# Attention and two expert stages on one core: block sums of the first two pairs by TensorE, two buffers for raw keys and queries, the other sums in three chunks on GpSimd

## Chip, core and metric

The kernel runs on one core of one Trainium2 chip. The metric is the device time of one execution in microseconds (us), as the median of several runs. Before the change it is 567.54 us (three runs, 567.53 to 567.76).

## What is computed

```python
# attention: B, H, S, D = 2, 8, 768, 64
block, window = (32, 16)
k_sum = k.reshape(B, H, nb, block, D).max(axis=3)      # nb = 24 blocks
v_sum = v.reshape(B, H, nb, block, D).mean(axis=3)
scores_l = scale * q @ k.T, kept where |i - j| < window
scores_s = scale * q @ k_sum.T + log(block)
a = softmax(concat([scores_l, scores_s], -1))
attn = a @ concat([v, v_sum])
# x = attn rows (1536 x 512); each row goes to one of 8 experts
out1[mask] = gate_w[mask, None] * (np.maximum(x[mask] @ w1[e], 0.0) @ w2[e])
# and then through a second layer
h = np.maximum(out1 @ w_in, 0.0)
out = h * h @ w_out
```

The change touches only the way to `v_sum` and the buffers of raw keys and queries. `v_sum` is 24 block means of the values for each of the 16 heads.

## The kernel before

The program is written for each engine by itself; the order in each engine's queue is the order in the text, and the engines meet by counting semaphores. Attention goes by pairs of heads: eight pairs, written as (it, par) with pair = 2 it + par. A pair's 768 queries are cut into 12 windows of 64 (SUBS); each window sees 94 near keys (NEAR) and the 24 block sums. A pair is done in two halves, g = 0 and 1, and the text numbers them n = 2 pair + g.

For one pair, SyncE loads raw keys and queries (`load_qk`, line 347) into `k_raw` and `q_raw`, a single buffer each, after the previous pair's were regrouped. VectorE regroups keys (`regroup_k`, 1326), ScalarE queries (`regroup_q`, 1099). TensorE turns them in three parts (`fill`, 701), the other engines move them out of PSUM (`move_k`, `move_kq`, `move_q`), VectorE takes the maximum of the key blocks (`key_max`) and TensorE makes the scores (`scores`, 715, 723, 730). ScalarE takes exponentials (`exps`, 1110). TensorE turns the probabilities (`turn_probs`, 743) and multiplies them with the value tile `v_win` (`values`, 763). `pair_step` on each engine (TensorE 781, ScalarE 1124, VectorE 1374) writes out how these interleave: while one pair is finished, the next one is scored and the one after that is turned.

A value tile `v_win` has 120 rows for each of the 12 windows: 94 near rows, loaded by `load_near` (361; six small-row DMAs on SyncE, 363, 364, 366), two unused ones and, in rows 96 to 119, the 24 block means, the same for all 12 windows. There are four tiles: 0 and 1 for even and odd pairs, 2 and 3 for the last two pairs. Their constant parts are cleared once: tiles 0 and 1 by VectorE (1445 to 1449), 2 and 3 by GpSimd (528 to 532).

The means come from `v_blk`, the values as 384 rows (one a block) of 32 x 64 in three chunks of 128 rows. The first chunk serves pairs 0, 1 and part of 2; half of it is added up by GpSimd (519), the other by VectorE (`sum_blocks`, 1431). SyncE stores its sums to `mean_dram` (391), waits, and loads them with a broadcast over the 12 windows into tiles 0 and 1 (378). Chunks 1 and 2 are added up by GpSimd (564, 567), which stores them itself (568). For pairs 2 to 7 SyncE loads the means into window 0 alone (373) and GpSimd copies them to the other eleven (599), counted by `means_spread`; it does that after its chunks and after its small constants (570 to 585).

After the pairs come the routing, gathers by GpSimd, the experts (`three`, lines 915 to 917) and the second layer (the same lines), all ordered behind the attention.

## Time and profile before

| | |
|---|---|
| median of three runs | 567.54 us |
| the profiled execution | 567.62 us |
| its span, first to last instruction | 565.9 us |
| mean granted TensorE clock | 0.969 |
| TensorE busy | 526.7 us, 93% |
| VectorE busy | 275.9 us, 49% |
| ScalarE busy | 236.0 us, 42% |
| GpSimd busy | 94.5 us, 17% |
| chain that ended last, by engine | PE 80%, DMA 5%, SPq 4%, DVE 4%, ACT 3% |

The profile is of one execution. PE is TensorE, PEld its weight loads, DVE VectorE, ACT ScalarE, POOL GpSimd, SPq the queue of SyncE. A busy share is a mean over stages with different limits. The chain is followed back from the last instruction, at each step to what released it; it says which work set the end. "issue" is time in which an engine waited for nothing that the profile shows. Helpers make several instructions share one line.

### The profile page before, as it was taken

Reading aid. Unit: us, or ns where it says so; the run is one execution under the profiler, and the core shown is the slowest. Engines: PE = TensorE matmul, PEld = TensorE weight load, DVE = VectorE, ACT = ScalarE, POOL = GpSimd, SP = SyncE. Lnnn points to the kernel's source line nnn. Section 1 sums busy time; section 2 is a strip of 40 time slices with the busy share of each in tenths; the row PEclk is TensorE's granted clock in tenths of the full one; section 3 lists DMA queues with packets and bytes.
Section 4 is the critical chain, followed back from the end, with each engine's and each line's share of the span. In section 5 each row is a group of like instructions: output and inputs, shape, how many; then the busy total and the mean of one; then the engine's idle time right before and its main releaser. Section 6 shows DMA issues by size and latency. Waiting matters only on the chain.

```text
span 565.9 us, 10958 instructions
## 1 busy us (share of the span) xinstructions
PE 526.7 (93%) x4442; PEld 475.2 (84%) x4442; DVE 275.9 (49%) x439; ACT 236.0 (42%) x416; POOL 94.5 (17%) x123
## 2 busy tenths in 40 slices
PE   5599987599999995999999999999999999999997
PEld 4487776598998985898989999889989999999995
DVE  7577867567675877465483232223223233222221
ACT  5478757455666652444452222223123222222221
POOL 5771111102653057211010000000000000000000
PEclk9689989699999999899999999999999999999999
DMA  6955776965769857385420020002002002000000
GB/s 204 273 165 153 188 205 215 294 230 164 284 223 350 287 182 259 131 286 190 175 76 0 1 75 1 0 13 62 0 0 74 0 0 74 0 0 37 2 2 37
DMA packets 62655, 69.50 MB, mean 123 GB/s; under 512 B 22512, under 2 KB 47088, under 8 KB 62232
## 3 DMA queue, kind: packets, MB, share of 16 engines
q1 hardware_dynamic: 59160, 57.36, 31.9%
q0 software_dynamic: 3456, 11.60, 6.0%
q8 instruction: 27, 0.44, 0.3%
q14 instruction: 12, 0.10, 0.1%
HBM read 58.88 MB, written 10.06 MB: 122 GB/s over the span
## 4 chain that ended last, share of the span: by engine, by line
PE 80%; DMA 5%; SPq 4%; DVE 4%; ACT 3%; issue 2%; POOL 2%; POOLq 0%; ACTq 0%; DVEq 0%
PE psum L915 24%; PE psum L916 23%; PE psum L917 23%; PE psum L701 1%; DMA k_raw<-in_k 1%; DMA x_rows_sb<-x_rows,gather_tab 1%; SPq L364 1%; PE psum L743 1%; PE psum L909 1%; DMA x_rows_sb<-x_rows,idx_g 1%; SPq L363 1%; PE psum L723 1%; PE psum L1018 1%; PE psum L763 1%; ACT prob L1110 1%
## 5 line engine op out<-in xcount | busy, mean ns | idle before, releaser
L917 PE MATMUL psum<-x_hi,win_lo 128*128 128x256 f32 x384 | 108.7, 283 | 0.0
L916 PE MATMUL psum<-x_lo,win_hi 128*128 128x256 f32 x384 | 108.7, 283 | 0.0
L915 PE MATMUL psum<-x_hi,win_hi 128*128 128x256 f32 x384 | 108.5, 282 | 0.0
L1722 DVE TENSOR_TENSOR h_sq<-h_relu 128x512 f32<-128x512 f32 x48 | 33.2, 693 | 126.5 <-ACT h_relu L1291 126.5
L915 PE MATMUL psum<-wb_hi,h_hi 128*128 128x512 f32 x208 | 83.2, 400 | 0.0
L1291 ACT ACTIVATE h_relu<-psum 128x512 f32<-128x512 f32 x48 | 28.7, 598 | 127.3 <-PE psum L917 127.3
L916 PE MATMUL psum<-wb_lo,h_hi 128*128 128x512 f32 x208 | 81.6, 392 | 0.0
L917 PE MATMUL psum<-wb_hi,h_lo 128*128 128x512 f32 x208 | 81.6, 392 | 0.0
L915 PEld LDWEIGHTS psum<-x_hi,win_hi 128*128 128x128 f32 x384 | 73.6, 192 | 1.4
L916 PEld LDWEIGHTS psum<-x_lo,win_hi 128*128 128x128 f32 x384 | 73.6, 192 | 1.4
L917 PEld LDWEIGHTS psum<-x_hi,win_lo 128*128 128x128 f32 x384 | 73.6, 192 | 0.0
L915 PE MATMUL psum<-x_hi,wa_hi 128*128 128x256 f32 x224 | 64.7, 289 | 0.6 <-DVE x_lo L1635 0.6
L916 PE MATMUL psum<-x_lo,wa_hi 128*128 128x256 f32 x224 | 64.1, 286 | 0.0
L917 PE MATMUL psum<-x_hi,wa_lo 128*128 128x256 f32 x224 | 64.1, 286 | 0.0
L1624 DVE TENSOR_TENSOR wa_lo<-w_raw,wa_hi 128x1024 fp32r<-128x1024 f32 x32 | 41.1, 1342 | 36.0 <-ACT wa_hi L1204 36.0
L1725 DVE TENSOR_TENSOR h_lo<-h_sq,h_hi 128x512 fp32r<-128x512 f32 x48 | 33.3, 693 | 33.0 <-ACT h_hi L1296 33.0
L917 PEld LDWEIGHTS psum<-wb_hi,h_lo 128*128 128x128 f32 x208 | 39.3, 189 | 8.5
L1296 ACT CAST h_hi<-h_sq 128x512 fp32r<-128x512 f32 x48 | 29.8, 620 | 40.0 <-DVE h_sq L1722 40.0
L915 PEld LDWEIGHTS psum<-wb_hi,h_hi 128*128 128x128 f32 x208 | 39.6, 190 | 7.6 <-issue 0.2
L916 PEld LDWEIGHTS psum<-wb_lo,h_hi 128*128 128x128 f32 x208 | 39.6, 190 | 7.3
L915 PEld LDWEIGHTS psum<-x_hi,wa_hi 128*128 128x128 f32 x224 | 43.7, 195 | 1.5 <-issue 1.2
L916 PEld LDWEIGHTS psum<-x_lo,wa_hi 128*128 128x128 f32 x224 | 43.8, 195 | 0.2
(211 smaller groups left out, 886.6 us busy)
## 6 DMA issues: line engine op xcount, KB each, us to landing
w_raw<-in_moe_w SPq DMA_DIRECT2D x56, 512.0 KB, 6.1
win_raw<-in_moe_w_in POOLq DMA_DIRECT2D x8, 512.0 KB, 7.2
w_raw<-in_moe_w_out SPq DMA_DIRECT2D x8, 512.0 KB, 4.8
k_raw<-in_k SPq DMA_DIRECT2D x8, 384.0 KB, 4.3
q_raw<-in_q SPq DMA_DIRECT2D x8, 384.0 KB, 4.6
v_blk<-in_v SPq DMA_DIRECT2D x3, 1024.0 KB, 7.5
v_win<-in_v SPq DMA_DIRECT2D x16, 192.0 KB, 3.5
x_rows<-x_all SPq DMA_DIRECT2D x8, 384.0 KB, 5.8
```

The source lines that it names most:

```text
L363: sp.dma_start(dst[PAD:PAD + QS, :, hh, 0:D], src[:, 0, :, :]).then_inc(v_loaded[slot], 16)
L364: sp.dma_start(dst[0:PAD, 1:SUBS, hh, 0:D], src[QS - PAD:QS, 0, 0:SUBS - 1, :])\
L701: mm = pe.transpose(psum[:, bank, n * P:(n + 1) * P], side[:, j, :, :].rearrange("p h d -> p (h d)"), ident[:, :])
L723: pe.matmul(ps_score[g][QS * s:QS * s + QS, hh, t, 0:SUM0], q_t[par][h0:h0 + D, i * QS:(i + 1) * QS], k_t[par][h0:h0 + D, i * QS:i * QS + ...
L915: pe.matmul(o, l_hi, r_hi, start=start, stop=False)
L916: pe.matmul(o, l_hi, r_lo, start=False, stop=False)
L917: return pe.matmul(o, l_lo, r_hi, start=False, stop=stop)
L1291: act.activation(h_relu[c % 2][:, :], ps_h[:, c % 4, :], ACT.Relu).then_inc(relu_made, 1)
L1296: act.copy(h2_hi[c % 3][:, :, :].rearrange("p f t -> p (f t)"), h_sq[c % 2][:, :])\
L1624: dve.tensor_tensor(lo[:, at:at + PIECE], w_raw[:, c, :], hi[:, at:at + PIECE], ALU.subtract)\
L1722: dve.tensor_tensor(h_sq[c % 2][:, :], h_relu[c % 2][:, :], h_relu[c % 2][:, :], ALU.mult)\
L1725: dve.tensor_tensor(h2_lo[c % 3][:, :, :].rearrange("p f t -> p (f t)"), h_sq[c % 2][:, :], h2_hi[c % 3][:, :, :].rearrange("p f t -> p (f ...
```

## The change

For pairs 0 and 1 TensorE makes the block sums from the near rows of the value tile: `sum_means` multiplies, window by window, a matrix `picks` of zeros and ones with the 94 near rows and adds the 12 products up in PSUM; VectorE copies the 24 sums into window 0 of the tile (`place_means`), and GpSimd copies them to the others, as it does for later pairs. The other six pairs' sums are made by GpSimd alone in three chunks of 96 rows (VB), the first of them between the spreads of pairs 0 and 1. The broadcast load is gone. GpSimd also clears tile 1 and regroups the keys of pair 1. Raw keys and queries have a second buffer, in the place of `x_all` slots that are written late. The order at the start of each engine's program is changed to match; all products with values now wait for their own pair's `means_spread`.

```diff
         v_heads = v.rearrange("b h (i r) d -> r (b h) i d", r=QS)
-        v_blocks = v.rearrange("b h (n t) d -> (b h n) (t d)", t=BLOCK).rearrange("(c p) x -> p c x", p=P)
+        v_blocks = v.rearrange("b h (n t) d -> (b h n) (t d)", t=BLOCK).rearrange("(c p) x -> p c x", p=VB)
...
+        def raw(pair):
+            if pair % 2 == 0:
+                return k_raw[:, :, :, :], q_raw[:, :, :, :]
+            return [x_all[:, i, :, :].rearrange("p t c -> p (t c)").rearrange("p (h j d) -> p h j d", h=2, j=TILES)
+                    for i in (PAIRS - 1, PAIRS - 2)]
...
             def load_qk(pair):
-                for dst, src, loaded, copied in ((k_raw, k_heads, k_loaded, k_regrouped),
-                                                 (q_raw, q_heads, q_loaded, q_regrouped)):
-                    if not (isinstance(pair, int) and pair == 0):
-                        sp.wait_ge(copied, pair)
-                    sp.dma_start(dst[:, :, :, :].rearrange("p h j d -> p h (j d)"),
-                                 src[:, bass.ds(2 * pair, 2), :]).then_inc(loaded, 16)
+                for dst, src, loaded, copied in ((raw(pair)[0], k_heads, k_loaded, k_regrouped),
+                                                 (raw(pair)[1], q_heads, q_loaded, q_regrouped)):
+                    if pair >= 2:
+                        sp.wait_ge(copied, pair - 1)
+                    sp.dma_start(dst.rearrange("p h j d -> p h (j d)"),
+                                 src[:, bass.ds(2 * pair, 2), :]).then_inc(loaded[pair % 2], 16)
...
                 slot = v_slot(it, par)
-                if it > 0:
-                    sp.dma_start(v_win[slot][SUM0:COLS, 0, :, 0:D], mean_heads[:, 4 * it + 2 * par:4 * it + 2 * par + 2, :])\
-                      .then_inc(means_loaded[slot], 16)
-                    return
-                for hh in range(2):
-                    mean = mean_heads[:, bass.ds(4 * it + 2 * par + hh, 1), :]
-                    sp.dma_start(v_win[slot][SUM0:COLS, :, hh, 0:D], mean.broadcast_to([NSUM, SUBS, D]))\
-                      .then_inc(v_loaded[slot], 16)
+                sp.dma_start(v_win[slot][SUM0:COLS, 0, :, 0:D], mean_heads[:, 4 * it + 2 * par:4 * it + 2 * par + 2, :])\
+                  .then_inc(means_loaded[slot], 16)
+            def load_blocks(c):
+                sp.dma_start(v_blk[0:VB, c - 1, :], v_blocks[:, c, :]).then_inc(vb_loaded[c - 1], 16)
             sp.dma_start(emb_sb[:, :], emb).then_inc(emb_loaded, 16)
             load_qk(0)
-            sp.dma_start(v_blk[:, 0, :], v_blocks[:, 0, :]).then_inc(vb_loaded[0], 16)
-            sp.dma_start(tau_sb[:, 0:1], tau.broadcast_to([P, 1])).then_inc(tau_loaded, 16)
+            load_qk(1)
             sp.wait_ge(zeros_made, 1)
             load_near(0, 0, free=True)
-            load_qk(1)
-            sp.wait_ge(zeros_made, 2)
+            sp.dma_start(tau_sb[:, 0:1], tau.broadcast_to([P, 1])).then_inc(tau_loaded, 16)
+            load_qk(2)
+            sp.wait_ge(late_zeros_made, 1)
             load_near(0, 1, free=True)
-            sp.wait_ge(mean_made, 1)
-            sp.dma_start(mean_dram[0:P, :], v_mean[:, 0, :]).then_inc(means_stored[0], 16)
-            sp.dma_start(v_blk[:, 1, :], v_blocks[:, 1, :]).then_inc(vb_loaded[1], 16)
-            sp.wait_ge(means_stored[0], 16)
-            load_means(0, 0)
-            load_means(0, 1)
-            load_qk(2)
-            sp.dma_start(v_blk[:, 2, :], v_blocks[:, 2, :]).then_inc(vb_loaded[2], 16)
+            load_blocks(1)
             load_qk(3)
-            sp.wait_ge(late_zeros_made, 1)
-            sp.wait_ge(means_stored[1], 16)
+            load_blocks(2)
             for it in range(1, PAIRS // 2 - 1):
                 for par in range(2):
                     load_near(it, par)
-                    if it == 1 and par == 1:
-                        sp.wait_ge(means_stored[2], 16)
+                    sp.wait_ge(means_stored[it - 1], 16)
                     load_means(it, par)
                     load_qk(2 * it + 2 + par)
+                    if it == 1 and par == 0:
+                        load_blocks(3)
+            sp.wait_ge(late_zeros_made, 3)
+            sp.wait_ge(means_stored[PAIRS // 2 - 2], 16)
             for par in range(2):
                 load_near(PAIRS // 2 - 1, par, free=True)
                 load_means(PAIRS // 2 - 1, par)
...
-            pool.wait_ge(vb_loaded[0], 16)
+            after(pool.memset(picks[:, :], 0.0))
+            pick = picks[:, SUBS * 2:SUBS * 2 + 2]
+            after(pool.memset(pick, 1.0))
+            after(pool.affine_select(out=pick, in_=pick, compare_op=ALU.is_ge, fill=0.0, base=-PAD,
+                                     pattern=[[-BLOCK, 2]], channel_multiplier=1))
+            pool.affine_select(out=pick, in_=pick, compare_op=ALU.is_ge, fill=0.0, base=PAD + BLOCK - 1,
+                               pattern=[[BLOCK, 2]], channel_multiplier=-1).then_inc(picks_made, 1)
+            pool.wait_ge(picks_made, 1)
             pool.wait_ge(consts_made, 1)
-            at = BLOCK * D // 2
-            width = at // 2
-            while width >= D:
-                last = pool.tensor_tensor(v_blk[:, 0, at:at + width], v_blk[:, 0, at:at + width],
-                                          v_blk[:, 0, at + width:at + 2 * width], ALU.add)
-                if width > D:
-                    after(last)
-                width //= 2
-            last.then_inc(half_summed, 1)
-            pool.wait_ge(half_summed, 1)
-            for i in range(2, 4):
+            pool.wait_ge(k_regrouped, 1)
+            pool.wait_ge(k_loaded[1], 16)
+            pool.sem_inc(pool_waited, 1)
+            pool.tensor_copy(k_side[1][:, :, :, :].rearrange("p j h d -> p h j d"), raw(1)[0]).then_inc(k_regrouped, 1)
+            pool.wait_ge(k_regrouped, 2)
+            def zero_windows(i):
                 pool.memset(v_win[i][:, 0, :, :], 0.0)
                 after(pool.memset(v_win[i][:, SUBS - 1, :, :], 0.0))
                 after(pool.memset(v_win[i][QS:SUM0, :, :, :], 0.0))
                 after(pool.memset(v_win[i][0:SUM0, :, :, D:D + 1], 1.0))
                 after(pool.memset(v_win[i][SUM0:COLS, :, :, D:D + 1], float(BLOCK)))
-            pool.sem_inc(late_zeros_made, 1)
+                pool.sem_inc(late_zeros_made, 1)
+            def sum_blocks(c):
+                pool.wait_ge(vb_loaded[c], 16)
+                pool.sem_inc(pool_waited, 1)
+                width = BLOCK * D // 2
+                while width > D:
+                    after(pool.tensor_tensor(v_blk[0:VB, c, 0:width], v_blk[0:VB, c, 0:width],
+                                             v_blk[0:VB, c, width:2 * width], ALU.add))
+                    width //= 2
+                after(pool.tensor_tensor(v_mean[0:VB, c, :], v_blk[0:VB, c, 0:D], v_blk[0:VB, c, D:2 * D], ALU.add))
+                pool.dma_start(mean_dram[(c + 1) * VB:(c + 2) * VB, :], v_mean[0:VB, c, :])\
+                    .then_inc(means_stored[c], 16)
+            def spread(at):
+                pool.tensor_copy(v_win[at][SUM0:COLS, 1:SUBS, :, 0:D],
+                                 v_win[at][SUM0:COLS, 0:1, :, 0:D].broadcast_to([NSUM, SUBS - 1, 2, D]))\
+                    .then_inc(means_spread, 1)
+            zero_windows(1)
+            pool.wait_ge(means_placed, 1)
+            spread(0)
+            pool.wait_ge(means_spread, 1)
+            sum_blocks(0)
+            pool.wait_ge(means_placed, 2)
+            spread(1)
+            pool.wait_ge(means_spread, 2)
+            zero_windows(2)
+            zero_windows(3)
...
             for c in (1, 2):
-                pool.wait_ge(vb_loaded[c], 16)
-                width = BLOCK * D // 2
-                while width > D:
-                    after(pool.tensor_tensor(v_blk[:, c, 0:width], v_blk[:, c, 0:width],
-                                             v_blk[:, c, width:2 * width], ALU.add))
-                    width //= 2
-                after(pool.tensor_tensor(v_mean[:, c, :], v_blk[:, c, 0:D], v_blk[:, c, D:2 * D], ALU.add))
-                pool.dma_start(mean_dram[c * P:(c + 1) * P, :], v_mean[:, c, :]).then_inc(means_stored[c], 16)
+                sum_blocks(c)
...
-                    if 2 * it + par > 2:
-                        pool.wait_ge(means_spread, 2 * it + par - 2)
-                        end_waits()
+                    pool.wait_ge(means_spread, 2 * it + par)
+                    end_waits()
                     pool.wait_ge(means_loaded[at], 16 if at > 1 else 16 * it)
-                    pool.tensor_copy(v_win[at][SUM0:COLS, 1:SUBS, :, 0:D],
-                                     v_win[at][SUM0:COLS, 0:1, :, 0:D].broadcast_to([NSUM, SUBS - 1, 2, D]))\
-                        .then_inc(means_spread, 1)
+                    spread(at)
...
-            def fill(it, par, f, bank=7, first=False):
+            def fill(it, par, f, bank=7):
                 pair = 2 * it + par
                 if f == 0:
                     pe.wait_ge(k_regrouped, pair + 1)
-                    if not first:
+                    if pair > 0:
                         pe.wait_ge(qk_moved_act, 2 * pair)
                 elif f == 1:
                     pe.wait_ge(q_regrouped, pair + 1)
-                    if not first:
+                    if pair == 1:
+                        pe.wait_ge(emb_moved, 1)
+                    elif pair > 1:
                         pe.wait_ge(qk_moved_act, 2 * pair + 1)
-                elif not first:
+                elif pair == 1:
+                    pe.wait_ge(qk_moved_act, 3)
+                elif pair > 1:
                     pe.wait_ge(qk_moved_dve, pair + 1)
                 tiles = [("k", j) for j in range(TILES)] + [("q", j) for j in range(TILES)]
...
             def values(it, par, g):
                 n = 2 * (2 * it + par) + g
-                if isinstance(n, int) and n == 0:
-                    pe.wait_ge(emb_moved, 1)
                 if g == 0:
                     last_two = v_slot(it, par) > 1
-                    pe.wait_ge(v_loaded[v_slot(it, par)], 96 if last_two else 128 + 96 * it)
-                    if it > 0:
-                        pe.wait_ge(means_spread, 2 * it + par - 1)
+                    pe.wait_ge(v_loaded[v_slot(it, par)], 96 if last_two else 96 * it + 96)
+                    pe.wait_ge(means_spread, 2 * it + par + 1)
...
+            def sum_means(par, bank):
+                pe.wait_ge(v_loaded[par], 96)
+                for i in range(SUBS):
+                    mm = pe.matmul(ps_mean(bank), picks[:, 2 * (SUBS - i):2 * (SUBS - i) + EP],
+                                   v_win[par][0:NEAR, i, :, 0:D], start=(i == 0), stop=(i == SUBS - 1))
+                mm.then_inc(means_summed, 1)
...
                 if pair > 0:
                     turn_pair(pair - 1)
+                else:
+                    sum_means(1, 4)
                 if fills:
                     fill(it + 1, par, 1)
                 if pair > 0:
                     wait_turned(pair)
+                else:
+                    pe.wait_ge(means_placed, 2)
                 turn_probs(it, par, 1)
...
             pe.wait_ge(consts_made, 1)
             scores(0, 0, 0, first=True)
+            fill(0, 1, 0)
+            fill(0, 1, 1, bank=6)
             scores(0, 0, 1, first=True)
-            for f in range(3):
-                fill(0, 1, f)
+            fill(0, 1, 2)
+            pe.wait_ge(picks_made, 1)
+            pe.wait_ge(qk_moved_dve, 2)
+            sum_means(0, 6)
             pair_step(0, 0, True)
...
             move_k(0, 0, first=True)
             move_q(0, 0, bank=5)
-            exps(0, 0, 0, first=True)
             regroup_q(0, 1, first=True)
             move_k(0, 1, first=True)
+            exps(0, 0, 0, first=True)
             move_q(0, 1)
             pair_step(0, 0, True, first=True)
...
+                else:
+                    place_means(1, 4)
                 if fills:
                     move_kq(it + 1, par)
...
+            def place_means(par, bank):
+                dve.wait_ge(means_summed, par + 1)
+                dve.tensor_copy(v_win[par][SUM0:COLS, 0, :, 0:D],
+                                ps_mean(bank)[0:NSUM, :].rearrange("p (h d) -> p h d", h=2)).then_inc(means_placed, 1)
+            dve.memset(v_win[0][:, 0, :, 0:D], 0.0)
+            dve.memset(v_win[0][:, SUBS - 1, :, 0:D], 0.0)
+            dve.memset(v_win[0][QS:SUM0, 1:SUBS - 1, :, 0:D], 0.0)
+            dve.memset(v_win[0][0:SUM0, :, :, D:D + 1], 1.0)
+            dve.memset(v_win[0][SUM0:COLS, :, :, D:D + 1], float(BLOCK)).then_inc(zeros_made, 1)
+            embeddings()
             regroup_k(0, 0, first=True)
-            embeddings()
             move_kq(0, 0, first=True, bank=4)
...
             row_max(0, 0, 1)
-            regroup_k(0, 1, first=True)
-            move_kq(0, 1, first=True)
             key_max(0, 1)
+            place_means(0, 6)
             pair_step(0, 0, True, between=invert_tau)
             pair_step(0, 1, True)
             pair_step(1, 0, True)
```

## Rows read from the trace of the kernel before

**Rows 1.** The page, part 1: busy us (share of the span) xinstructions.

```profile
PE 526.7 (93%) x4442; PEld 475.2 (84%) x4442; DVE 275.9 (49%) x439; ACT 236.0 (42%) x416; POOL 94.5 (17%) x123
```

**Rows 2.** Chain of waits, 0 to 90 us: start us, length us, what.

```profile
17.38 2.03 DMA mean_rows<-v_mean
...
39.47 3.02 DMA k_raw<-in_k
...
46.26 0.99 ACT k_t L1082
...
52.65 0.90 issue
...
59.14 0.58 PE psum L701 x4
...
76.98 1.08 PE psum L701 x4
```

**Rows 3.** Timeline of GpSimd: start, length (us), line, operation, count [idle before <- releaser].

```profile
6.20 0.11 POOL L512 MEMSET mask<- 128x15 bf16 x1
11.07 3.38 POOL L519 TENSOR_TENSOR v_blk<-v_blk 128x512 f32<-128x512 f32 x4 [4.77 <-DMA v_blk<-in_v]
14.52 0.23 POOL L528 MEMSET v_win<- 120x160 f32 x1
...
19.62 0.13 POOL L531 MEMSET v_win<- 96x24 f32 x1
19.81 0.13 POOL L532 MEMSET v_win<- 24x24 f32 x1
23.12 5.24 POOL L564 TENSOR_TENSOR v_blk<-v_blk 128x1024 f32<-128x1024 f32 x4 [3.18 <-DMA v_blk<-in_v]
...
29.83 5.09 POOL L564 TENSOR_TENSOR v_blk<-v_blk 128x1024 f32<-128x1024 f32 x4
35.00 0.32 POOL L567 TENSOR_TENSOR v_mean<-v_blk 128x64 f32<-128x64 f32 x1
...
36.54 0.22 POOL L570 MEMSET ones<- 128x128 f32 x1
...
38.11 0.25 POOL L585 TENSOR_SCALAR_AFFINE_SELECT before<-id_e 48x48 f32<-48x48 f32 x1
41.30 1.36 POOL L599 COPY v_win<-v_win 24x1408 f32<-24x1408 f32 x1 [2.94 <-DMA v_win<-mean_rows]
49.26 1.36 POOL L599 COPY v_win<-v_win 24x1408 f32<-24x1408 f32 x1 [6.60 <-DMA v_win<-mean_rows]
```

**Rows 4.** Timeline of TensorE, 0 to 90 us.

```profile
17.14 1.11 PE L701 MATMUL psum<-ident,k_side 128*128 128x128 f32 x4 [5.52 <-DVE k_side L1326]
...
27.88 0.92 PE L763 MATMUL psum<-v_win,prob_t 120*64 120x65 f32 x24
...
37.07 0.92 PE L763 MATMUL psum<-v_win,prob_t 120*64 120x65 f32 x24
...
45.20 0.92 PE L763 MATMUL psum<-v_win,prob_t 120*64 120x65 f32 x24
...
50.24 0.92 PE L763 MATMUL psum<-v_win,prob_t 120*64 120x65 f32 x24
...
54.81 0.92 PE L763 MATMUL psum<-v_win,prob_t 120*64 120x65 f32 x24
```

**Rows 5.** Timeline of the queue of SyncE.

```profile
7.60 3.13 SPq L364 DMA_DIRECT2D v_win<-in_v  x1
...
12.20 1.56 SPq L363 DMA_DIRECT2D v_win<-in_v  x1
...
17.83 0.43 SPq L392 DMA_DIRECT2D v_blk<-in_v  x1
```

**Rows 6.** Timeline of VectorE, 0 to 90 us.

```profile
51.58 0.56 DVE L1326 COPY k_side<-k_raw 128x768 f32<-128x768 f32 x1 [1.19 <-DMA k_raw<-in_k]
```

**Rows 7.** Busy time by stretch; PEclk (granted clock) stands before the DMA share.

```profile
77.00:80.40 3.40, 3.40 (x46) 3.05 (x46) 2.10 (x4) 1.66 (x7) 1.36 (x1) 0.51 0.94 278
```

More of the change, by code:

```diff
@@ L55 @@
 PAIRS2 = F2 // P // 2
+VB = 2 * 2 * NSUM
 WARM = 14
@@ L152, in build @@
         slot_id = sb("slot_id", [P, HB], scope=one)
-        sb("filler", [P, (96256 - 95000) // 4], scope=one)
+        picks = sb("picks", [NEAR, SUBS * 2 + EP], scope=one)
+        sb("filler", [P, (96256 - 95000) // 4 - SUBS * 2 - EP], scope=one)
         hots = ExitStack()
@@ L235, in build @@
         before_made = sem("before_made")
-        k_loaded = sem("k_loaded")
-        q_loaded = sem("q_loaded")
+        k_loaded = [sem(f"k_loaded{i}") for i in range(2)]
+        q_loaded = [sem(f"q_loaded{i}") for i in range(2)]
         k_regrouped = sem("k_regrouped")
@@ L1095, in regroup_q @@
                 pair = 2 * it + par
-                act.wait_ge(q_loaded, 16 * (pair + 1))
+                act.wait_ge(q_loaded[par], 16 * (pair // 2 + 1))
                 if not first:
                     act.wait_ge(qk_filled, 3 * pair - 3)
-                act.copy(q_side[par][:, :, :, :].rearrange("p j h d -> p h j d"), q_raw[:, :, :, :])\
+                act.copy(q_side[par][:, :, :, :].rearrange("p j h d -> p h j d"), raw(pair)[1])\
                    .then_inc(q_regrouped, 1)
@@ L1458, in _ @@
             row_max(0, 0, 0)
-            sum_blocks()
+            move_kq(0, 1, first=True, bank=6)
             row_max(0, 0, 1)
-            regroup_k(0, 1, first=True)
-            move_kq(0, 1, first=True)
             key_max(0, 1)
+            place_means(0, 6)
             pair_step(0, 0, True, between=invert_tau)
```

32 lines of the change are left out of this document (9 added, 23 removed).

## The prediction

> **What bounds the kernel now.** I read the page first. TensorE is busy 93% of the span and the expert stages are nearly solid, so no early saving is lost or gained there; the open time is in the first 90 us, the attention [rows 1]. The chain of waits comes next, because it says which engine ends last in each part [rows 2]. Up to 28 us it is SyncE's queue and DMA: value tiles are issued, block means go to DRAM and back, and the single raw key buffer is refilled late. A second such piece ends with the key load from 39.47 us, which releases VectorE at 42.5 us. From there on, the chain goes only between ScalarE, TensorE and VectorE: softmax exponentials, regrouping of queries, transposes, the product with the values. So from about 43 us the attention is bound by its engines, and whatever delays one pair there delays the end.
>
> The third view is GpSimd's own timeline, because the change gives it most of its new work [rows 3]. Today it halves the first block sum with VectorE (3.38 us), clears two value windows (14.52 to 19.94 us), waits 3.18 us for a load, sums two chunks (23.12 to 36.54 us), makes constants (to 38.36 us), waits 2.94 us for the means of the third pair and then spreads them over its value windows (41.30 to 42.66 us). The fourth view is where TensorE stands: its product with the values, line 763, starts at 45.20 us for the third pair (pair 2 in the code) and at 54.81 us for the next [rows 4]. Each pair has two such products, numbered n = 0, 1, 2 and so on; n = 4, the third pair's first, is the one to watch. Its spread is finished 2.5 us before it.
>
> **Removed.** The 1 MB load of the first v_blk, VectorE's part of its sum and GpSimd's (3.38 us), the store of the means (2.03 us in the chain) and four broadcast loads behind it leave the front [rows 2, 3]. Raw keys and queries of pair 1 are asked for at about 2.3 us (third in SyncE's queue, where the v_blk load stood) instead of behind the first value tile, so the 5.52 us in which TensorE waited for them up to 17.14 us mostly goes [rows 4]. My estimate for n = 0 is 18 us instead of 27.88 us: scores of pair 0 end near 12.9 us as transposes of pair 1 are put between them, the sums for pair 0 follow, then the probability transposes and scores of pair 0/1. This saving is real, but it stands ahead of the wait that I find below, so it only decides how long TensorE then stands.
>
> **Added on TensorE and VectorE.** Twelve 94x32 by 128-column products for each of two pairs. No row has this shape. From below: the 65-column value products take 0.92 us for 24, 38 ns each, so 0.5 us for twelve. From above: the 128-column transposes at their slowest, 1.08 us for four, give 3.2 us. I take the same transposes at the full clock, 0.58 us for four, so 1.8 us a pair, since the columns are as many [rows 2, 4]. The copies out of PSUM (24x128) cost VectorE less than its copy of 768 columns, 0.56 us [rows 6]. All of it lies before 25 us. A pair_step of pair 0 now also waits for the value tile of pair 1 to land (its last issue is near 17.5 us, landing some 2 to 3 us later) before the sums and the second probability transposes; behind that wait in TensorE's queue stand scores, transposes and n = 1. That costs a few us at about 20 us, again ahead of the later wait.
>
> **Added on GpSimd, step by step.** The mask is done at 6.31 us. The picks matrix is two memsets and two selects of at most 56 columns, by the rows of small ones (0.11 to 0.25 us) 0.8 us. The key copy of 768 columns takes 0.75 us by the spread (1.36 us for 1408) and up to 1.8 us by the adds (5.1 us for some 1,900), once the keys have landed near 7.5 us (2.3 us and the 5.2 us that the 1 MB load from 17.83 us took) [rows 3, 5]. Clearing window 1 takes 2.7 us (half of 5.42). So the wait for late_zeros_made ends at 11.5 to 12.5 us, about when SyncE gets there: nothing or 0.5 us. Spread of pair 0, 1.4 us, is done by 18 us. The next step is sum_blocks(0), and its load is issued only behind the value tile of pair 1. That tile takes SyncE about 5 us (12.20 us to shortly before 17.83 us now, [rows 5]); with the queue in the new order I put it at 12.3 to 17.5 us and the load at 17.5 us. Today the one issued at 17.83 us released GpSimd at 23.12 us [rows 3, 5]. It is 3/4 of the size, but has a larger key and query load ahead of it. I take 22.5 us, with 21 and 25 us as ends.
>
> What one sum costs: GpSimd starts the first at 23.12 us and the second at 29.83 us, so 6.71 us with its semaphores and the store's issue; the second takes 6.71 us as well, 29.83 to 36.54 us [rows 3]. The chunks shrink from 128 to 96 partitions, and there are three of them instead of two and a shared one. Does GpSimd's time shrink with partitions? The rows say no: a 96x24 memset and a 24x24 one both took 0.13 us [rows 3]. The Trainium skill ("GPSIMD Engine Reference", § 2.1 Instruction dispatch) says the same: eight cores take the same instruction, each for its own 16 partitions. By its § 3.1 a two-input add costs 2.6 cycles a column at 1.2 GHz, so as an estimate 4.4 us for the 2048 columns of a sum; here its five instructions and the gaps between them took 5.5 to 5.6 us (5.09 + 0.08 + 0.32 for the second), and the measurement decides. By the page's price the delay below would be about 3 us smaller.
>
> So, in GpSimd's order: 22.5 + 6.7 (sum) = 29.2; spread of pair 1, 1.4, to 30.6; windows 2 and 3, 5.4, to 36.0; two more sums, 13.4, to 49.4; the small constants, 1.86, to 51.3; and only then the spread of pair 2, 1.36, to 52.6 us. Semaphores add some 0.2 us. The product n = 4 waits for means_spread 3, which is this one. **It starts at 52.8 us instead of 45.20 us, 7.6 us later.** In between TensorE stands: pair 1's values can start at 30.8 us (37.07 us today), n = 3 follows at about 35 us, and n = 4 would be ready near 40 us. SyncE does not gate this: the last chunk is issued after the means of chunk 1 are stored (about 33 us) and lands near 40 us, before GpSimd asks for it at 42.7 us.
>
> **What the delay becomes at the end.** After n = 4 the chain was of engines alone [rows 2], so it is carried on. Added to it: TensorE comes out of some 12 us of idleness. After the short wait up to 76.98 us its granted clock was 0.51 for 3.4 us (so 1.2 of 2.4 GHz) [rows 7], and four transposes took 1.08 us in the chain against 0.58 us at the full clock [rows 2]. In the step from n = 4 to n = 5 (5.0 us today, 45.20 to 50.24 us) part of this falls on time in which it waits for VectorE anyway; I take +1.0 us, between 0 and 2.5. Against it: the raw buffers are double, so VectorE's wait for keys at 51.58 us (1.19 us) goes, and the stall of 0.9 us for issue inside a row of score products at 52.65 us may go with it [rows 2, 6]. I take -0.5 us, between 0 and -1. Later spreads have room: the one for n = 6 ended at 50.6 us for a product at 54.81 us [rows 3, 4]. Together 7.6 + 1.0 - 0.5 = 8.1 us. The profiled execution took 567.62 us at a span of 565.9 us, the median of the three runs is 567.54 us. 567.6 + 8.1 = 575.7; I give 575.6 us, a loss of 1.4%.
>
> **Rivals.** (a) GpSimd still decides, but the delay is smaller, 2.5 to 5 us, so 570 to 572.5 us: the first chunk lands by 18 us, or a sum costs 3/4 with 96 partitions (5.0 us, three times 1.7 us less: 7.6 - 5.1 = 2.5 us). For it: chunk 1 is smaller, the queue lighter. Against: partition counts change nothing in the rows, and even with no wait for the load at all, GpSimd's work after the spread of pair 0 at about 17.7 us is 30.1 us, which ends at 47.8 us, 2.6 us after today's start. 13%.
> (b) The delay is larger, 580 to 584 us: the load is late as near-tile descriptors back SyncE up (one issue took 3.13 us already, [rows 5]), the clock stays low for the whole next pair, or the sums wait for VectorE. 9%.
> (c) Faster: GpSimd is not what n = 4 waits for. The point from which it decides is the end of its spread: if that comes before about 40 us, the gain of the front (37.07 - 31 = 6 us, n = 2) is carried on instead, and the time is 562 us. For this the price of the three sums (20 us) would have to fall by 13 us, to about a third. For it speaks only that no row shows a sum with VectorE idle. 4%.
> (d) No difference: the front's gain shows up after n = 4 through work done ahead (ScalarE's and VectorE's queues empty while they stand), giving 7 us back. Against: the pair took 9.6 us between its first product and the next pair's, 0.9 us of it the stall [rows 2, 4]. 3%. That the change does not do what it says would be the old DRAM way for pairs 0 and 1 still waited for; the diff leaves no such wait, so it has no share.
>
> **Chances and range.** The forecast's own case (573 to 580 us) has 71%, (a) 13, (b) 9, (c) 4, (d) 3. The range 571 to 580 us holds all of the first and about two thirds of (a), some 80%. Faster by more than 0.2% 0.04, within 0.2% 0.03, slower 0.93; 0.2% (1.1 us) is about what a measurement of this kernel can tell from no change.
>
> **What would show each step.** Right: TensorE's value product of pair 0 near 18 us and of pair 1 near 31 us, released by GpSimd's spread; three groups of sums on GpSimd of 6.7 us each with chunk 1 starting at 21 to 25 us; the third spread starting at about 51 us straight after the constants with no wait for its load; TensorE idle over 10 us before the third pair, then a granted clock of 0.5; the stages after it shifted by the same 8 us to the end. Wrong: a sum well under 6 us; GpSimd waiting again for means before the third spread, which would mean that it is not late; or TensorE's distance from n = 4 to the first expert product shrinking by more than 2 us.

## The result

The changed kernel takes 574.52 us (median of four runs, 571.68 to 575.42), the kernel before 567.59 us (four runs): a ratio of 1.0113, with a 95% interval of 1.0078 to 1.0148. It is slower, by 6.9 us. The profiled execution of after took 574.73 us, with a span of 573.0 us, 7.1 us more than that of before. From chip to chip and run to run both kernels move by some us (the kernel before had medians of 569.33, 566.97 and 567.59 us in the three later batches), so below a ratio is always to the kernel before on the same chip at the same time.

The page of after: head, busy times, two rows of the 40 slices, and the chain by engine.

```profile
span 573.0 us, 11063 instructions
...
PE 535.5 (93%) x4490; PEld 483.7 (84%) x4490; DVE 270.6 (47%) x430; ACT 236.3 (41%) x416; POOL 102.9 (18%) x137
...
POOL 6487010112373238310010000000000000000000
PEclk9995999589999999799999999999999999999999
...
PE 84%; issue 5%; DVE 5%; DMA 4%; ACT 2%; POOL 1%; POOLq 0%; ACTq 0%; DVEq 0%
```

TensorE is busy 8.8 us longer and has the same share as in [rows 1]. A slice is 14.3 us; the fourth (43 to 57 us) has a granted clock of 5 tenths. The chain no longer shows a share for SyncE's queue, which had 4%.

GpSimd's timeline in after, from the key copy to the spread of the third pair (pair 2); it answers to [rows 3]:

```profile
7.94 0.82 POOL L533 COPY k_side<-x_all 128x768 f32<-128x768 f32 x1 [0.19 <-POOL picks L525]
...
19.76 1.36 POOL L557 COPY v_win<-v_win 24x1408 f32<-24x1408 f32 x1 [8.39 <-DVE v_win L1480]
22.39 5.04 POOL L549 TENSOR_TENSOR v_blk<-v_blk 96x1024 f32<-96x1024 f32 x4 [1.27 <-DMA v_blk<-in_v]
...
28.93 1.36 POOL L557 COPY v_win<-v_win 24x1408 f32<-24x1408 f32 x1
30.35 0.24 POOL L537 MEMSET v_win<- 120x160 f32 x1
...
36.19 5.25 POOL L549 TENSOR_TENSOR v_blk<-v_blk 96x1024 f32<-96x1024 f32 x4 [0.28 <-POOL v_win L541]
...
44.01 5.01 POOL L549 TENSOR_TENSOR v_blk<-v_blk 96x1024 f32<-96x1024 f32 x4 [1.34 <-DMA v_blk<-in_v]
...
50.22 0.22 POOL L600 MEMSET ones<- 128x128 f32 x1
...
51.81 0.25 POOL L615 TENSOR_SCALAR_AFFINE_SELECT before<-id_e 48x48 f32<-48x48 f32 x1
52.31 1.36 POOL L557 COPY v_win<-v_win 24x1408 f32<-24x1408 f32 x1 [0.25 <-POOL before L615]
```

The three sums are the groups of line 549 (each in four wide adds, and a fifth that is not shown), the spreads the copies of 24x1408. The spread of pair 2 is the last line: it ends at 53.67 us, where before it ended at 42.66 us.

TensorE in after, which answers to [rows 4]: line 809 is the sums, 732 the transposes, 791 the values.

```profile
16.55 2.81 PE L809 MATMUL psum<-v_win,picks 94*32 94x128 f32 x24
...
22.18 0.92 PE L791 MATMUL psum<-v_win,prob_t 120*64 120x65 f32 x24
...
33.57 0.92 PE L791 MATMUL psum<-v_win,prob_t 120*64 120x65 f32 x24
...
38.41 0.92 PE L791 MATMUL psum<-v_win,prob_t 120*64 120x65 f32 x24
...
43.35 0.23 PE L761 MATMUL psum<-k_max,q_t 64*64 64x24 f32 x1 [2.45 <-issue]
...
44.07 1.11 PE L732 MATMUL psum<-ident,k_side 128*128 128x128 f32 x4
53.77 1.57 PE L791 MATMUL psum<-v_win,prob_t 120*64 120x65 f32 x24 [8.59 <-issue]
...
59.92 0.92 PE L791 MATMUL psum<-v_win,prob_t 120*64 120x65 f32 x24
...
63.21 0.92 PE L791 MATMUL psum<-v_win,prob_t 120*64 120x65 f32 x24
```

The values of pair 0 start 5.7 us earlier than in [rows 4], those of pair 1 3.5 us earlier. Then TensorE has its transposes done at 45.18 us, stands for 8.59 us, and starts n = 4 at 53.77 us, 0.1 us after the spread. The trace names no releaser there, only "issue"; that it is the spread is what the experiments show. Where the 7.1 us arise:

| stretch | before | after | difference |
|---|---|---|---|
| start to n = 4 | 45.20 | 53.77 | +8.57 |
| n = 4 to n = 5 | 5.04 | 6.15 | +1.11 |
| n = 5 to the first gather (95.58, 102.36) | 45.34 | 42.44 | -2.90 |
| first gather to the end of the span | 470.32 | 470.64 | +0.32 |

The stretches of the granted clock show where the second row comes from. After the times and counts, the columns at the end are clock, DMA share, GB/s:

```profile
45.00:50.00 5.00, 0.18 (x1) 0.00 (x0) 0.08 (x1) 1.06 (x1) 4.39 (x6) 0.50 0.54 163
50.00:55.00 5.00, 1.23 (x23) 1.26 (x24) 0.00 (x0) 0.00 (x0) 4.51 (x14) 0.50 0.03 8
55.00:60.00 5.00, 4.99 (x81) 4.29 (x79) 3.78 (x8) 2.42 (x8) 0.19 (x1) 0.78 0.00 0
```

### The profile page after: what moved, and what is told of

Read it like the earlier page. It is cut to its first block, busy times and chain, and to the rows that moved or that the text cites. A ratio compares the mean times of both kernels' runs of the same rounds, so it can differ in the third digit from the quotient of the medians.

```text
span 573.0 us, 11063 instructions
## 1 busy us (share of the span) xinstructions
PE 535.5 (93%) x4490; PEld 483.7 (84%) x4490; DVE 270.6 (47%) x430; ACT 236.3 (41%) x416; POOL 102.9 (18%) x137
## 4 chain that ended last, share of the span: by engine, by line
PE 84%; issue 5%; DVE 5%; DMA 4%; ACT 2%; POOL 1%; POOLq 0%; ACTq 0%; DVEq 0%
PE psum L959 23%; PE psum L960 23%; PE psum L961 23%; PE psum L732 3%; PE psum L791 2%; PE psum L774 2%; PE psum L754 1%; DMA x_rows_sb<-x_rows,gather_tab 1%; DMA x_rows_sb<-x_rows,idx_g 1%; PE psum L953 1%; PE psum L809 1%; PE psum L1062 1%; DVE wb_lo L1661 1%; PE psum L801 1%; PE psum L761 1%
## 5 line engine op out<-in xcount | busy, mean ns | idle before, releaser
L1661 DVE TENSOR_TENSOR wa_lo<-w_raw,wa_hi 128x1024 fp32r<-128x1024 f32 x32 | 42.6, 1389 | 36.9 <-ACT wa_hi L1248 36.9
L961 PEld LDWEIGHTS psum<-wb_hi,h_lo 128*128 128x128 f32 x208 | 39.5, 190 | 8.5
```

The lines of the kernel that those rows point to most:

```text
L961: return pe.matmul(o, l_lo, r_hi, start=False, stop=stop)
L1661: dve.tensor_tensor(lo[:, at:at + PIECE], w_raw[:, c, :], hi[:, at:at + PIECE], ALU.subtract)\
```

## The experiments

The theory is that GpSimd's queue decides: the spread of pair 2 stands behind two sums that pair 2 does not need. The rivals are that the new front costs (the products of sums on TensorE, the new waits), and, from the trace of after, that the stall of 2.45 us for issue at 40.9 us does. Below, a time and a ratio are of several runs; starts and ends are of the one that was profiled.

**e1_order: the order on GpSimd alone.**

```diff
+            def spread_next(it, par):
+                at = v_slot(it, par)
+                pool.wait_ge(means_spread, 2 * it + par)
+                end_waits()
+                pool.wait_ge(means_loaded[at], 16 if at > 1 else 16 * it)
+                spread(at)
+
+            spread_next(1, 0)
+            sum_blocks(1)
+            spread_next(1, 1)
+            sum_blocks(2)
-            for c in (1, 2):
-                sum_blocks(c)
...
-            for it in range(1, PAIRS // 2):
+            for it in range(2, PAIRS // 2):
```

> Nothing is left out; on GpSimd the spreads of pairs 2 and 3 go ahead of the second and third sum. If GpSimd's queue order is the cause (my theory), the spread of pair 2 ends near 37.5 us, n = 4 starts at 42 to 45 us instead of 53.77, and the kernel takes 563 to 567 us, faster than both. If the cost lies in the changed front itself (products of sums on TensorE, more waits, the spreads for pairs 0 and 1), it stays at 571 us or more.

Measured: 562.74 us, a ratio of 0.9882 (0.9831 to 0.9933). GpSimd's timeline of e1_order (549 is the sums):

```profile
37.72 1.70 POOL L557 COPY v_win<-v_win 24x1408 f32<-24x1408 f32 x1 [0.26 <-POOL v_win L541]
39.49 5.00 POOL L549 TENSOR_TENSOR v_blk<-v_blk 96x1024 f32<-96x1024 f32 x4
...
45.80 1.36 POOL L557 COPY v_win<-v_win 24x1408 f32<-24x1408 f32 x1
47.23 5.25 POOL L549 TENSOR_TENSOR v_blk<-v_blk 96x1024 f32<-96x1024 f32 x4
```

and TensorE's at the same place:

```profile
43.23 0.23 PE L766 MATMUL psum<-k_max,q_t 64*64 64x24 f32 x1 [3.00 <-issue]
...
44.68 1.57 PE L796 MATMUL psum<-v_win,prob_t 120*64 120x65 f32 x24
```

Nothing but the place of two spreads has changed, and the kernel goes from 1.1% slower to 1.2% faster. The spread of pair 2 is finished 5.3 us before n = 4, so n = 4 has other waits. Of the front nothing was taken away, so its new work cannot be what made the change slow. At n = 4 only 0.5 us of the front's gain is left (44.68 against 45.20 us), behind a stall of 3.00 us for issue. From n = 4 to n = 5 this run lost 1.0 us against the kernel before, and from there to the first gather it gained 3.2 us, where from 75 to 85 us its granted clock was 1.00 and the kernel before had its 3.4 us at 0.51 [rows 7]. So part of its gain is the clock's; e9_order_twin, with a granted clock of 0.72 from 74 to 80 us, is still 0.5% faster than the kernel before.

**e2_before_busy: the delay alone, in the kernel before.**

```diff
+            for _ in range(2):
+                width = BLOCK * D // 2
+                while width >= D:
+                    after(pool.tensor_tensor(v_blk[:, 1, 0:width], v_blk[:, 1, 0:width],
+                                             v_blk[:, 1, width:2 * width], ALU.add))
+                    width //= 2
             pool.memset(ones[:, :], 1.0)
```

> The kernel before, with ten more adds on GpSimd after its two sums (about 11.2 us by 5.6 us for five; they add up values that nothing reads afterwards, the output stays whole). By my theory a late spread of pair 2 is enough: it moves from 41.3 to about 49.7 us, n = 4 from 45.20 to 51.3 us, and the time is 567.6 + 6.1 + 1.1 for the clock = 574 to 575 us, as slow as the changed kernel without any of the change. If GpSimd has slack there, it stays at 567.6 us.

Measured: 573.57 us, 1.0091 (1.006 to 1.0123). GpSimd and TensorE of e2_before_busy:

```profile
38.06 11.20 POOL L573 TENSOR_TENSOR v_blk<-v_blk 128x1024 f32<-128x1024 f32 x10
...
51.30 1.35 POOL L606 COPY v_win<-v_win 24x1408 f32<-24x1408 f32 x1 [0.16 <-POOL before L592]
```

```profile
43.24 0.92 PE L770 MATMUL psum<-v_win,prob_t 120*64 120x65 f32 x24
...
52.76 1.57 PE L770 MATMUL psum<-v_win,prob_t 120*64 120x65 f32 x24 [5.64 <-POOL v_win L606]
```

Here the trace names the releaser: TensorE sat 5.64 us until GpSimd's spread. n = 4 came at 52.76 us and not at 51.3 us as expected, because GpSimd waited longer for its two chunks (their sums started at 24.06 and 31.71 us, in the kernel before at 23.12 and 29.83 us). 11.2 us of adds that nobody reads cost the old kernel as much as the change does, on the same chip as e4_after_again with its 1.0111.

**e3_fewer_adds: a smaller dose in the changed kernel.**

```diff
-                width = BLOCK * D // 2
+                width = BLOCK * D // 4
```

> The changed kernel with the widest add (1024 columns, 2.4 us) of all three sums left out, so that half of each block is not in the means. GpSimd's work before the spread of pair 2 falls by 7.2 us, but the last chunk's load, now landing at 44.0 us, may take its place; I expect the spread to start at 47 to 49 us instead of 52.3, n = 4 at 48.5 to 50.5, and 569 to 572 us. If GpSimd does not decide, 574.5 us stays.

Measured: n = 4 at 50.98 us, just after the end of the spread at 50.88 us. The whole time, 547.38 us (0.9616), can't be compared: half of each block is missing from the means, so the results and with them the routing are others, and TensorE has 152 products fewer than in after (4338 against 4490). GpSimd of e3_fewer_adds:

```profile
37.20 0.53 POOL L553 DMA_DIRECT2D mean_rows<-v_mean  x1 [0.31 <-POOL v_mean L552]
43.67 2.58 POOL L549 TENSOR_TENSOR v_blk<-v_blk 96x512 f32<-96x512 f32 x3 [5.93 <-DMA v_blk<-in_v]
...
49.53 1.35 POOL L557 COPY v_win<-v_win 24x1408 f32<-24x1408 f32 x1 [0.25 <-POOL before L615]
```

Taking out 7.2 us of adds brought 2.8 us at this place, because the last chunk's load released GpSimd only at 43.67 us, after 5.93 us of waiting. The expectation was off by half a us at n = 4: the load is close behind the adds as the next limit.

**e4_after_again** is the changed kernel unchanged, for its spread.

> The changed kernel once more, for its spread from run to run. The four times so far lie between 571.68 and 575.42 us. I expect n = 4 at 53.8 us again within 0.5 us, and if the total differs, that it comes from stalls for issue in the row of TensorE's products or from a stretch at the lower granted clock near 85 us, of which the profiled run had few.

Measured: 575.44 us, 1.0111 (1.006 to 1.0163). n = 4 started at 52.66 us, 1.1 us earlier than in after and not within the half us expected, the first gather at 103.22 us, 0.9 us later. Between them n = 4 to n = 5 took 7.16 us instead of 6.15, and the granted clock was 0.66 from 85 to 90 us, where after had 1.00. So the attention behind n = 4 varies by 2 us from run to run, by the clock. That n = 4 came earlier is the last chunk: its load was issued at 33.71 us instead of 35.28 us, and GpSimd, which took it up at 42.90 us, did not wait for it.

**e5_chunk_early: the last chunk's load issued at 18 to 20 us, on top of e1_order.**

```diff
             load_blocks(2)
+            load_blocks(3)
...
-                    if it == 1 and par == 0:
-                        load_blocks(3)
```

> Nothing is left out. As e1_order, and the load of the last chunk is issued at about 18 us behind the second one instead of at about 35 us. In e1_order TensorE stood 3.0 us for issue at 40.2 to 43.2 us, where the DMA engines were 0.9 to 1.0 busy; in the changed kernel 2.45 us, in e3_fewer_adds, which issued that load earlier, 0.25 us. If that stall comes from the load, it falls below 1 us, n = 4 starts near 42.5 us instead of 44.7, and the time falls by 1 to 2.5 us against e1_order, to 560.5 to 562 us. If the stall belongs to the place in the program, n = 4 stays at 44 to 45 us and the time at 562.7.

Measured: 562.82 us, 0.9911 (0.9867 to 0.9956). TensorE's value products in e5_chunk_early:

```profile
32.52 0.92 PE L795 MATMUL psum<-v_win,prob_t 120*64 120x65 f32 x24 [1.38 <-issue]
...
37.59 0.92 PE L795 MATMUL psum<-v_win,prob_t 120*64 120x65 f32 x24
...
43.06 0.92 PE L795 MATMUL psum<-v_win,prob_t 120*64 120x65 f32 x24 [1.05 <-DVE x_all L1415]
```

n = 4 at 43.06 us as expected, with no stall for issue at 41 us. VectorE waited 3.25 us for its keys instead, to 40.73 us. The time is above the 560.5 to 562 us expected; the median is that of e1_order (on another chip), so this run alone shows no gain. The 1.38 us ahead of n = 2 are no stall for issue, though the trace calls them so. GpSimd's spread of pair 1 in e5_chunk_early:

```profile
31.06 1.35 POOL L556 COPY v_win<-v_win 24x1408 f32<-24x1408 f32 x1
```

It ended at 32.41 us, and n = 2 started at 32.52 us. The same 0.1 us stands in e6, e7 and e9 (spread to 31.94, 31.42 and 32.31 us, n = 2 at 32.05, 31.52 and 32.41 us, after waits of 2.56, 1.34 and 2.02 us). So n = 2 has the fault of n = 4: the spread of pair 1 stands behind the first sum, which it does not need, and that sum waits for its load. No run puts it ahead of that sum.

**e6_single_raw: waits as with one raw buffer, on top of e1_order.**

```diff
-                        sp.wait_ge(copied, pair - 1)
+                        sp.wait_ge(copied, pair)
```

> As e1_order, but keys and queries of a pair are only asked for when the previous pair's have been regrouped, as with one buffer. If the second raw buffer carries much of the front's gain, n = 2 moves from 32.9 to 35 us or later, and the time rises by 2 to 3 us to about 565 us. If TensorE's sums alone carry it, it stays within 1 us of e1_order.

Measured: 563.23 us, 0.9929 (0.9877 to 0.9981); n = 2 at 32.05 us, n = 4 at 45.77 us. n = 2 did not move back; it even stood 2.56 us for the spread of pair 1. n = 4 is 1.1 us later than in e1_order, behind a stall of 3.28 us for issue. The time is within 1 us of e1_order's, so the double buffering of later pairs shows nothing clear of the noise; the early load of pair 1, which this kernel keeps, was not taken out.

**e7_windows_later: clearing windows 2 and 3 behind the second sum, on top of e5_chunk_early.**

```diff
-            zero_windows(2)
-            zero_windows(3)
...
             sum_blocks(1)
+            zero_windows(2)
+            zero_windows(3)
```

> As e5_chunk_early, and GpSimd clears windows 2 and 3 behind its second sum instead of before the spread of pair 2, so that spread can end near 36 us and VectorE's key copy at 31 us meets no clearing. In e1_order that copy took 1.06 us, in the changed kernel 1.98 us with the clearing beside it, elsewhere 0.56 us. By my account GpSimd is no longer what n = 4 waits for in e1_order (its spread ends at 39.4 us, n = 4 starts at 44.7), so n = 4 moves by at most 0.5 us and the time stays within 0.7 us of e5_chunk_early. If GpSimd still decides, it gains 2 us or more.

Measured: 564.45 us, 0.9938 (0.9895 to 0.9981). n = 4 at 44.05 us, 1.0 us later than in e5_chunk_early where I expected 0.5 at most; its spread of pair 2 ended at 39.5 us, after waiting for its means. VectorE's key copy at 28.93 us took 0.55 us as expected. The time is 1.6 us above e5_chunk_early on the same chip, not within 0.7, though the intervals overlap. The trace shows where n = 4 lost its 1 us. VectorE's next key copy and GpSimd's second sum in e7_windows_later:

```profile
39.97 2.32 DVE L1374 COPY k_side<-k_raw 128x768 f32<-128x768 f32 x1 [3.52 <-DMA k_raw<-in_k]
```

```profile
39.53 5.21 POOL L548 TENSOR_TENSOR v_blk<-v_blk 96x1024 f32<-96x1024 f32 x4
```

The copy began beside the sum's first add (39.53 to 41.86 us) and took 2.32 us; TensorE waited 3.00 us for it. In e5_chunk_early the same copy began at 40.73 us, before the add at 40.96 us, and took 0.56 us. The spread was not what n = 4 waited for, as the theory had it; but GpSimd delayed it in another way (see the last section).

**e8_half_order: the spread of pair 2 between the second and the third sum** (the lines are against e1_order).

```diff
+            sum_blocks(1)
             spread_next(1, 0)
-            sum_blocks(1)
             spread_next(1, 1)
```

> Nothing is left out. Between the changed kernel and e1_order: the spread of pair 2 stands behind the second sum, but before the third. It should end near 44.5 us (53.67 in the changed kernel, 39.42 in e1_order). If a late spread costs only beyond TensorE's own time, n = 4 starts at 44.7 to 46 us and the time is 563 to 565 us. If each us of GpSimd delay costs one us, it lies 5 us above e1_order, at 568.

Measured: 565.68 us, 0.9972 (0.9924 to 1.002). GpSimd's spread of pair 2 and TensorE's n = 4 and n = 5 in e8_half_order:

```profile
43.54 1.35 POOL L557 COPY v_win<-v_win 24x1408 f32<-24x1408 f32 x1
```

```profile
45.00 1.57 PE L796 MATMUL psum<-v_win,prob_t 120*64 120x65 f32 x24 [1.40 <-issue]
...
52.17 0.92 PE L796 MATMUL psum<-v_win,prob_t 120*64 120x65 f32 x24
```

The spread ended at 44.89 us, n = 4 came 0.1 us behind it: this is the knee, and TensorE stood 1.40 us for it. n = 4 is where I expected it. The time is 0.7 us above the upper end that I gave: after two stalls (2.45 us for issue, then the 1.40 us) TensorE ran at the lower clock (0.83 over 40 to 60 us, 1.00 in e5_chunk_early), and n = 4 to n = 5 took 7.17 us. How much of that the 1.40 us cost isn't shown: e6_single_raw, whose spread was early, had the same 0.83 over 40 to 60 us after a stall of 3.28 us for issue alone, and took 6.33 us.

**e9_order_twin and e10_chunk_early_twin** are e1_order and e5_chunk_early again, on one chip, ten runs each.

> The kernel of e1_order on the chip of e10 and e11, for the comparison: 0.988 to 0.992 of the kernel before, with a stall for issue of 2 to 3 us near 41 us and n = 4 at 44 to 45 us.

> The kernel of e5_chunk_early on the same chip. If the stall of 3.0 us that its early load removed near 41 us carries through to the end, it is 1 to 2 us below e9_order_twin. In the other view the early load only moves the stall forward (1.38 us near 31 us in e5_chunk_early), n = 4 keeps at most 1 us of it, and the two differ by less than 1 us.

Measured: 564.01 us, 0.9950 (0.9923 to 0.9976), and 562.75 us, 0.9910 (0.9880 to 0.9940). n = 4 stood at 42.69 and 41.10 us. The early load is 1.3 us lower, in the expected direction, but the intervals overlap. e9 lies outside the 0.988 to 0.992 that I expected and came nearer to the kernel before than e1_order did; the gain of this order is better given as 0.5 to 1.2% than by one run. In e9 the stall at 41 us was 0.66 us, not 2 to 3, so its length varies in one and the same program. The expectation for e10 took the 1.38 us of e5 for this stall moved forward; it was the wait for the spread of pair 1. The four profiles with the early load (e5, e7, e10, e11) have no stall there, the seven with the late one (after, e1, e3, e4, e6, e8, e9) have 0.25 to 3.28 us. That is a pattern that speaks for a tie between the stall and that load; what the load does to TensorE, and what sets the length, is not shown.

**e11_chunk_early_only: that load moved in the changed kernel, and nothing else.**

```diff
             load_blocks(2)
+            load_blocks(3)
```

> The changed kernel with the last chunk's load issued at about 18 us and nothing else. GpSimd's wait for it (1.34 us at 42.7 us) goes, the stall for issue near 41 us goes too, but n = 4 still waits for the spread of pair 2: I expect that to end at 52.3 us, n = 4 at 52.4, and the time 1 us or so below the changed kernel, 1.009 of the kernel before. If the stall and not GpSimd were the cost, the time would fall by 2.5 us or more.

Measured: 573.65 us, 1.0102 (1.0066 to 1.0137). TensorE in e11_chunk_early_only:

```profile
40.07 0.66 PE L731 MATMUL psum<-ident,k_side 128*128 128x128 f32 x4
53.21 1.57 PE L790 MATMUL psum<-v_win,prob_t 120*64 120x65 f32 x24 [12.48 <-issue]
```

The stall is gone, the transposes are done at 40.7 us, and TensorE then stands 12.48 us instead of 8.59. n = 4 starts at 53.21 us, 0.8 us later than expected: the first sum began 0.64 us later than in after (23.03 us), and the second took 0.2 us longer. The time did not fall by the 2.5 us that the stall would have given back. TensorE has to stand for GpSimd's spread with or without it, so the stall does not explain the loss, and the third theory falls.

| kernel | spread of pair 2 ends | n = 4 | n = 5 | first gather | ratio |
|---|---|---|---|---|---|
| before | 42.66 | 45.20 | 50.24 | 95.58 | 1 |
| after | 53.67 | 53.77 | 59.92 | 102.36 | 1.0113 |
| e4_after_again | 52.55 | 52.66 | 59.82 | 103.22 | 1.0111 |
| e11_chunk_early_only | 53.11 | 53.21 | 60.07 | 103.47 | 1.0102 |
| e2_before_busy | 52.65 | 52.76 | 59.19 | 102.36 | 1.0091 |
| e8_half_order | 44.89 | 45.00 | 52.17 | 95.58 | 0.9972 |
| e6_single_raw | 38.87 | 45.77 | 52.10 | 95.55 | 0.9929 |
| e7_windows_later | 39.45 | 44.05 | 50.90 | 94.93 | 0.9938 |
| e5_chunk_early | 40.87 | 43.06 | 48.45 | 90.36 | 0.9911 |
| e1_order | 39.42 | 44.68 | 50.69 | 92.84 | 0.9882 |
| e9_order_twin | 39.2 | 42.69 | 47.52 | 91.16 | 0.9950 |
| e10_chunk_early_twin | 38.5 | 41.10 | 46.12 | 89.24 | 0.9910 |

Where the spread ends after 44 us, n = 4 follows it by 0.1 us; where it ends before 43 us, n = 4 goes by other waits.

## Why the prediction was right, and where it was off

**The place of the limit was right.** I had the spread of pair 2 end at 52.6 us and n = 4 start at 52.8 us; they came at 53.67 and 53.77 us, and e1, e2 and e8 show from three sides that this wait makes the loss. The forecast of 575.6 us lies 1.1 us above the measured 574.52 us. Of the signs that I named, the third spread came straight after the constants with no wait for its load, and from n = 4 to the first expert product it is 60.84 us instead of 62.06 us, so less than 2 us shorter. TensorE's idle stretch before n = 4 was 8.59 us and not over 10, together with the stall for issue ahead of it 11.0 us.

**GpSimd's sum, term by term.** The first chunk released it at 22.39 us (22.5 forecast). A sum with its store took 6.54 us (22.39 to 28.93) and 6.21 us (44.01 to 50.22), where I took 6.7: 96 partitions cost what 128 did, so the price by partitions, my rival (a), is refuted. A 1024-column add took at most 2.36 us, against 2.38 us in the kernel before. Clearing two windows took 5.84 us (30.35 to 36.19) for 5.4, the constants to the spread 2.09 us for 1.86. The step that failed was the last load: I had it land near 40 us, ahead of its sum; it landed at 44.0 us, 8.6 us after its issue, and GpSimd waited 1.34 us for it. With 0.4 us more for the clearing, 0.2 us more for the constants and 1.0 us less for the start and the three sums, n = 4 is 1 us later than I wrote. In e4_after_again, the same program, GpSimd did not wait for this load and the spread ended at 52.55 us, so in that run the step held. A sum adds 1984 columns, not the 2048 that I counted beside it; the forecast goes by the measured sums and does not use this.

**TensorE's added work was mis-sized.** The sums of a pair took 2.81 us at a granted clock of 1.00, where I took 1.8 (between 0.5 and 3.2). The trace counts 24 products for the 12 in the text, 117 ns each. It does so for the values too: the 24 of [rows 4] are 12 in the text, so my 38 ns was half a product and the lower bound should have been 0.9 us. Pair 0's values came at 22.18 us, not 18 us. Most of that is not the sums, but their start at 16.55 us: TensorE's first transposes and scores took about twice as long as in the kernel before (six transposes of queries 1.49 us for 0.82 us), with a granted clock of 1.00 on record for the stretch. In e9_order_twin the same scores soon ran fast, the sums started at 13.79 us and pair 0's values at 19.41 us; why after's did not is open. Pair 1's values came at 33.57 us, not 31 us. Just before them TensorE stood 1.49 us for a key copy that took 1.98 us instead of 0.56 us, beside GpSimd's clearing, a cost that I had at nothing. None of this had an effect on the total, as it stands ahead of the long wait; it did set what rival (c) could bring. That rival's mechanism was right with the order changed, but its size wasn't: the front gives 3.5 us at n = 2 and, in e1_order, 0.5 us at n = 4; e1_order reached 562.74 us only with what the later stretch also gave back.

**The clock.** I took +1.0 us for n = 4 to n = 5, 1.11 us was measured (2.1 us in e4_after_again). The granted clock was 0.50 from 45 to 55 us, so 1.2 of 2.4 GHz, and n = 4 itself took 1.57 us instead of 0.92.

**What was given back was more than I took.** For everything after n = 5 I had -0.5 us; it was -2.9 us. From n = 5 to n = 6 it is 3.29 instead of 4.57 us, with the 0.90 us stall of [rows 2] gone. From n = 9 to n = 11 it is 11.04 instead of 13.60 us: there the kernel before had a stall of 0.70 us and the 3.4 us at a clock of 0.51 [rows 7], and after ran at 1.00. Two later steps were longer by 0.4 and 0.5 us (n = 7 to n = 8 and n = 11 to n = 12). The second part is luck of the run, as e4_after_again shows, which had a low stretch again (0.66 from 85 to 90 us) and gave back 1.9 us. So the total came out close partly because two misses offset each other: n = 4 was 1 us later than forecast and the rest 2.4 us shorter.

**The other rivals.** (b), 580 us and more, needed a late first chunk or a longer low clock; neither came. (d) had work done ahead give 7 us back; 2.9 us came back, through the stalls and the clock named above, and no run shows that work done ahead had a part in it.

## What to carry to other kernels

On an engine that runs its queue in order, sort work by when it is due, not by kind: here two sums and a row of constants stood ahead of a 1.4 us copy that needed none of them, and moving that copy turned 1.1% of loss into 0.5 to 1.2% of gain. When work is moved to a lightly loaded engine (17% busy), add up its queue from the last event it must wait for to the first result that somebody else waits for; the busy share says nothing about that. Such a wait can cost more than its length: after 5.6 to 12.5 us of it (e2, after, e4, e11) TensorE started at half the clock, and the step from n = 4 to n = 5 took 1.1 to 2.1 us more. A wait that the profile puts down to issue can be one for a semaphore: compare its end with the end of what the program says it needs, here 0.1 us apart in every case.

## What the runs showed of the hardware

VectorE's key copy of 768 columns takes 0.56 us alone and up to 2.32 us (in e7_windows_later, beside an add) when GpSimd works beside it. VectorE in after:

```profile
30.95 1.98 DVE L1370 COPY k_side<-x_all 128x768 f32<-128x768 f32 x1
...
59.79 0.56 DVE L1370 COPY k_side<-x_all 128x768 f32<-128x768 f32 x1
```

The first ran from 30.95 us, while GpSimd's memset of 1.69 us ran from 30.82 us; the same copy in e7_windows_later, with no clearing beside it, took 0.55 us. The kernel before shows the same once, VectorE and then GpSimd:

```profile
15.80 1.27 DVE L1326 COPY k_side<-k_raw 128x768 f32<-128x768 f32 x1 [0.19 <-DMA k_raw<-in_k]
```

```profile
14.97 1.69 POOL L530 MEMSET v_win<- 32x1920 f32 x1
```

The Trainium skill ("SBUF — State Buffer", § SBUF: two separate sides) calls the port pair that the two engines share an exclusive lock, under which the later one blocks. The trace agrees: both copies end about 0.4 us after the memset that they met (32.93 and 32.51 us, 17.07 and 16.66 us), the one in e7_windows_later 0.4 us after the add (42.29 and 41.86 us), as if nearly all of a copy had run only then. Where the copy came first, GpSimd was the one held up: in e1_order the spread at 37.72 us took 1.70 us instead of 1.36 us, beside a key copy from 37.63 to 38.19 us. It adds a price to work put on GpSimd that its own timeline does not show.

A 0.75 MB load of 8 KB rows took 8.6 us to land when issued at 35.28 us among value tiles, keys and queries (DMA share 0.87 over that time), and as little as 5.5 us in other runs (e10_chunk_early_twin). And TensorE can stall for up to 3.3 us for issue inside a row of score products that wait for nothing. The same program had 3.00 us once and 0.66 us the other time (e1_order, e9_order_twin); what sets the length was not settled.
